# Bucket attention and two dense layers: the order of early loads and of two roundings

## What is computed

```python
q_bits = (einsum('bhsd,dk->bhsk', q, proj) > 0)      # the same for k
q_bucket = sum(q_bits * 2 ** arange(6))              # a bucket number for each row
mask = q_bucket[:, :, :, None] == k_bucket[:, :, None, :]
scores = where(mask, q @ k.T / 8, -1e9)
x = softmax(scores) @ v                              # then 1536 tokens x 512
h = x @ w_in;  g = P(h) / (Q(h) + 1e-6);  y = g @ w_out      # 512 -> 2048 -> 512
h = y @ w_in2; g = h * relu6(h + 3) / 6;  out = g @ w_out2   # 512 -> 2048 -> 512
```

## Time and profile before

| | |
|---|---|
| median of 3 runs | 822.86 us (822.78 to 823.11) |
| profiled execution | 823.14 us, its span 821.3 us |
| PE busy | 766.7 us (93% of the span) |
| DVE, ACT, POOL busy | 479.0, 439.6, 223.3 us |
| chain that ended last | PE 85%, DMA 4%, ACT 3%, SP's queue 3% |
| mean granted clock of PE | 0.981 |

### The profile page before, as it was taken

How to read it: one execution, slowest core, us unless ns; L and a number is a source line. 1 busy time by engine, 2 the same in 40 slices (tenths; PEclk the granted TensorE clock), 3 DMA queues, 4 the chain that set the end, 5 groups by cost and what they waited for, 6 DMA issues and landing times.

```text
span 821.3 us, 11268 instructions
## 1 busy us (share of the span) xinstructions
PE 766.7 (93%) x3712; PEld 592.8 (72%) x3712; DVE 479.0 (58%) x793; ACT 439.6 (54%) x783; POOL 223.3 (27%) x364
## 2 busy tenths in 40 slices
PE   2689996887979999999999999999999999999998
PEld 1466665554656668888888888888888888888886
DVE  3577764555756668888988899984221322232223
ACT  1567665465656668987766689884222122212221
POOL 1455664554746514430000024443000000000000
PEclk9999997989989999999999999999999999999999
DMA  5634334333322013330000013331000100000001
GB/s 121 150 91 122 93 88 99 94 88 87 82 70 67 1 27 91 90 103 0 0 0 0 0 39 97 97 103 52 1 0 1 51 0 0 0 37 15 1 1 51
DMA packets 35372, 43.31 MB, mean 53 GB/s; under 512 B 4480, under 2 KB 23680, under 8 KB 35328
## 3 DMA queue, kind: packets, MB, share of 16 engines
q1 hardware_dynamic: 34752, 42.32, 19.4%
q10 hardware_dynamic: 576, 0.43, 0.2%
HBM read 26.61 MB, written 3.15 MB: 36 GB/s over the span
## 4 chain that ended last, share of the span: by engine, by line
PE 85%; DMA 4%; ACT 3%; SPq 3%; issue 2%; DVE 2%; ACTq 0%; POOL 0%; POOLq 0%; DVEq 0%
PE y_ps L912 32%; PE h_ps L858 11%; PE h_ps L859 11%; PE h_ps L860 11%; PE o_ps L838 6%; PE t_ps L821 6%; PE s_ps L811 4%; PE s_ps L812 3%; SPq L287 2%; DMA k_cross<-q_cross 2%; ACT probs L442 2%; DMA w_raw<-in_moe_w_in 2%; ACT q_main L436 1%; PE p_ps L795 1%; DMA bit_col<-bit_row 1%
## 5 line engine op out<-in xcount | busy, mean ns | idle before, releaser
L858 PE MATMUL h_ps<-x_hi,slot 128*128 (+1 forms) x384 | 149.7, 390 | 0.0
L859 PE MATMUL h_ps<-x_lo,slot 128*128 (+1 forms) x384 | 149.4, 389 | 0.0
L860 PE MATMUL h_ps<-x_hi,slot 128*128 (+1 forms) x384 | 149.4, 389 | 0.0
L704 DVE SCALAR_TENSOR_TENSOR t_abs<-t_abs,h_ps 128x512 f32<-128x512 f32 x48 | 33.0, 688 | 187.2 <-ACT t_abs L514 187.2
L401 POOL TENSOR_TENSOR slot<-w_raw,slot 128x512 fp32r<-128x512 f32 x64 | 81.8, 1295 | 206.9 <-ACT slot L469 206.7
L514 ACT ACTIVATE t_abs<-h_ps,three_col 128x512 f32<-128x512 f32 x48 | 33.1, 690 | 191.9 <-PE h_ps L860 191.9
L912 PE MATMUL y_ps<-g_hi,slot 128*128 128x512 f32 x384 | 126.1, 389 | 0.0
L442 ACT ACTIVATE probs<-s_ps,exp_bias,exp_scale 128x768 f32<-128x768 f32 x96 | 95.1, 991 | 52.0 <-POOL exp_bias L388 51.3
L612 DVE TENSOR_REDUCE neg_max<-s_ps 128x1 f32<-128x768 f32 x96 | 91.6, 954 | 52.6 <-PE s_ps L812 52.5
L912 PE MATMUL y_ps<-slot,g_hi 128*128 128x512 f32 x384 | 118.3, 389 | 0.0
L811 PE MATMUL s_ps<-k_cross,q_cross 128*128 128x512 f32 x192 | 79.6, 414 | 32.4 <-ACT probs L442 28.3
(11 more groups left out here) (71 smaller groups left out, 1173.0 us busy)
## 6 DMA issues: line engine op xcount, KB each, us to landing
w_raw<-in_moe_w_in SPq DMA_DIRECT2D x32, 256.0 KB, 2.7
w_raw<-in_moe_w_out SPq DMA_DIRECT2D x32, 256.0 KB, 2.7
raw<-in_q SPq DMA_DIRECT2D x17, 192.0 KB, 3.2
v_nat<-in_v SPq DMA_DIRECT2D x16, 192.0 KB, 2.5
raw<-in_k SPq DMA_DIRECT2D x15, 192.0 KB, 3.4
k_main<-q_main SPq DMA_DIRECT2D x15, 192.0 KB, 2.6
k_cross<-q_main SPq DMA_DIRECT2D x15, 192.0 KB, 3.1
k_cross<-q_cross SPq DMA_DIRECT2D x15, 192.0 KB, 2.6
```

The source lines that it names most:

```text
L858: mm(h_ps[b][:, :], w_hi, x_hi[:, kt, cols], start=(kt == 0), stop=False)
L859: mm(h_ps[b][:, :], w_hi, x_lo[:, kt, cols], start=False, stop=False)
L860: last = mm(h_ps[b][:, :], w_lo, x_hi[:, kt, cols], start=False, stop=(kt == KT - 1))
```

## The change

It does four things. The early weights of a pair are asked for right behind `load_v`, ahead of `place_head`. They are split in steps 7 and 10 instead of 4 and 8. The projection weights are the first DMA of both queues. The second copy of head 0 goes to `swapped`, which is `probs[3]`, so that `raw[1][0]` is free: `load_raw(1, 0)` stands right behind the loads of the first pair, `load_raw(1, 1)` behind the first bits, ahead of `place_head(1)`, and `load_v(0)` behind that.

```diff
-    EARLY_AT = (4, 8)
+    EARLY_AT = (7, 10)
...
+            swapped = probs[3]
...
+            sp.dma_start(proj_raw[0:D, :], proj).then_inc(proj_in, 16)
             sp.dma_start(raw[0][0][0:D, :], q_dram[dram_head(0, 0), :, :]).then_inc(raw_in[0][0], 16)
-            sp.dma_start(raw[1][0][D:P, :], q_dram[dram_head(0, 0), :, :]).then_inc(swapped_in, 16)
-            sp.dma_start(proj_raw[D:P, :], proj).then_inc(proj_in, 16)
+            sp.dma_start(swapped[D:P, :], q_dram[dram_head(0, 0), :, :]).then_inc(swapped_in, 16)
             load_raw(0, 1)
+            load_raw(1, 0)
             sp.wait_ge(bits_made, 1)
             sp.wait_ge(first_q, 2)
             place_bits(sp, 0, 0)
+            load_raw(1, 1)
+            place_head(1)
             load_v(0)
-            place_head(1)
-            sp.wait_ge(first_k, 2)
-            load_raw(1, 0)
-            load_raw(1, 1)
             load_raw(2, 0)
             load_raw(2, 1)
...
                 if u == 0 and i >= 1:
                     load_v(i)
+                if u == 0 and EARLY_PAIR <= i < EARLY_PAIR + EARLY_SLOTS:
+                    load_weights(0, i - EARLY_PAIR)
                 if h + 2 < NHEAD:
                     place_head(h + 2)
                 if h + 6 < NHEAD:
                     load_raw((h + 6) // 2, h % 2)
-                if u == 0 and EARLY_PAIR <= i < EARLY_PAIR + EARLY_SLOTS:
-                    load_weights(0, i - EARLY_PAIR)
...
+            act.dma_start(proj_raw[D:P, :], proj).then_inc(proj_in, 16)
             act.dma_start(raw[0][0][D:P, :], k_dram[dram_head(0, 0), :, :]).then_inc(raw_in[0][0], 16)
-            act.dma_start(proj_raw[0:D, :], proj).then_inc(proj_in, 16)
-            act.dma_start(raw[1][0][0:D, :], k_dram[dram_head(0, 0), :, :]).then_inc(swapped_in, 16)
+            act.dma_start(swapped[0:D, :], k_dram[dram_head(0, 0), :, :]).then_inc(swapped_in, 16)
```

More of the change, by code:

```diff
@@ L489, in _ @@
             for to in (k_main, k_cross):
-                nc.scalar.activation(to[0][0:D, :], raw[1][0][0:D, :], ACT.Copy).then_inc(first_k, 1)
+                nc.scalar.activation(to[0][0:D, :], swapped[0:D, :], ACT.Copy).then_inc(first_k, 1)
             act.wait_ge(bits_made, 1)
@@ L661, in _ @@
             dve.wait_ge(swapped_in, 32)
-            nc.vector.tensor_copy(q_cross[0][D:P, :], raw[1][0][D:P, :]).then_inc(first_q, 1)
+            nc.vector.tensor_copy(q_cross[0][D:P, :], swapped[D:P, :]).then_inc(first_q, 1)
             nc.vector.tensor_tensor(q_cross[0][0:D, :], raw[0][0][0:D, :], q_main[0][0:D, :].bitcast(F32),
```

## The result

The changed kernel takes 786.82 us (median of 4 runs, 786.21 to 787.28) against 822.99 us (822.78 to 823.25) for the kernel before, a ratio of 0.956 with a 95% interval of 0.9543 to 0.9577. Its span is 785.5 us, 35.8 less than before. The prediction was 787.5 us, a gain of 35.4; the medians differ by 36.2.

What follows compares the result with a forecast made beforehand. PE bounds pair 2; the early pairs lose time to a weight wait and lower clock, the beginning to late loads. 30.9 - 4.1 + 8.6 = 35.4 us gained, from 822.86 to 787.5 us, range 782.5 to 793.0.

Steps and rivals of the forecast that it cites:

- -30.9 us: Attention pairs 3 to 6: asking for early weights first removes the whole wait and the clock's fall, -30.9 us.
- +1.02 x 4 = +4.1 us: Early pairs: POOL's split in step 8 delays exponential 9, costing PE 1.02 us in each of four pairs.
- the 0.2 assumed: Early pairs: ACT's own split delays exponential 7 by some 0.2 us, for which PE does not wait.
- The price of the split in step 11: Early pairs: POOL's second split, moved from step 9 to 11, costs nothing, as POOL idles after odd steps.
- The term of 8.6 us: Beginning: pair 1's loads in front bring scores 2 8.8 us earlier, less 0.2 for company beside bit_col.
- Projection weights first ... worth nothing by itself: Start of both queues: two tiny DMAs moved ahead of raw[0][0] gain nothing, since first bits wait for bit_col.
- the rule cited from the Trainium skill: Beginning: transfers from different engines share 16 DMA engines and interleave; by it alone the gain is 6.5 instead of 8.6 us.
- Rivals 1 to 5: Split 8 hidden 783.4 (0.12); splits dearer 792.6 (0.13); late beginning 790.8 (0.10); weights late 814.3 (0.03); placing late 825.3 (0.01).
- rival 3: Beginning gives only its lower bound, 5.3 us, as bit_col or the second raw is late: 790.8 us, chance 0.10.

Runs made afterwards that it cites:

- the run with step 10: The changed kernel with splits in steps 7 and 9, so POOL's stand in steps 8 and 10: 787.52 us, ratio 0.9582.
- the run behind the bits: The changed kernel with load_raw(1, 0) behind the first bits, right ahead of load_raw(1, 1): 787.71 us, ratio 0.9585.
- the beginning alone: The changed kernel with the old order of the early weights and splits in steps 4 and 8: 816.06 us, ratio 0.9927.

## Why the prediction was right

**The wait.** -30.9 us was right: the order alone gave 30.85. It came from windows of equal work, with and without the wait, which also held what the fall of the clock cost. That both halves of the edit remove it independently was not in the prediction, though its numbers were: weights asked for 16.4 us behind the seam and at work 19.9 behind it, against step 7 at 19.0.

**The splits.** The place and the mechanism were right, shown by the run that moves POOL's split alone out of step 8 (the price goes) and the run that moves ACT's alone out of step 7 (it stays). The term "+1.02 x 4 = +4.1 us" measured 27.92 against 30.85, so 2.93 us, or 0.73 a pair. The delay itself measured 0.89; I took an exponential's start to the scores as 1.21 us, but that was a row behind the stall, at the low clock, and here it is 127.30 - 126.16 = 1.14. And I left out the 0.14 that PE gets back at the next tile. That ACT's own split does not delay PE was right; exponential 7 starts 19.56 us behind the seam against 19.54 in pair 2 before, even less than the 0.2 assumed. The price of the split in step 11, nothing, was right. Its reason, "an odd step, where POOL afterwards idles", was too narrow, as the run with step 10 shows.

**The beginning.** The term of 8.6 us measured 7.87, of which 7.16 stand at scores 2. The difference, by its own steps: `bit_col` came 1.02 us later, not 0.2, and the first key bits let scores 0 begin 5.97 us behind the first bits instead of 5.25, which I did not have at all. Scores 0 so began 1.74 us later. 13.59 us lay between scores 0 and scores 2 before and 4.69 now, so the middle part gave 8.90, and 8.90 - 1.02 - 0.72 = 7.16. The step that failed is "Projection weights first ... worth nothing by itself". With them back in their old places, and the extra `raw` still beside `bit_col`, the first bits are at 8.69 us again; this is one profiled execution, but it lies outside the 9.12 to 9.83 us of the seven profiled kernels that have them first and `bit_col` in its old place. I had looked for the cause in the extra `raw`, of which the run behind the bits (9.12, against 9.25 to 9.83) shows at most a part. Why two transfers of 1.5 KB ahead of two tiles cost `bit_col` a microsecond stays open.

The 0.72 us lie in the landing of the key bits. The second half of them is issued by ACT 2.3 us behind the start of the first bits both before (at 11.0 us) and after (at 12.0), and scores 0 follow 2.9 us behind that issue before and 3.7 after. From first bits to scores 0 it took 5.79 to 6.02 us in the nine other profiled kernels with a `raw` load of pair 1 issued right behind the first bits, and 5.25 to 5.48 in the three that load v there. That fits other company in the DMA engines. It is also the one place where the rule cited from the Trainium skill, "DMA: Bandwidth & Descriptors", section "Issuing engines are not separate DMA queues", would bear on the trace: these bits are issued by ACT and the tiles by SP. The trace is in line with it but does not show it, as the load at that point was not tried alone.

**The clock in pair 0.** The remaining 0.71 us are in no term. The prediction put a change of clock only at scores 2. The fall near 47 us, which the kernel before has and the changed one has not, was missed; the earlier trace rows do not show it either, as they dip only from 123 us on. The runs speak for chance: the two kernels that keep the old beginning (steps alone, order alone) have no such fall and take 51.22 us from scores 2 to the seam of pair 2, just as the changed kernel does. Over all profiled kernels this stretch took from 50.0 to 52.9 us with the same work. So a gain of a microsecond at the beginning can't be read from the total. And it was luck that the total came as close as it did: the beginning gave 7.16 us where 8.6 were forecast, and the cheaper splits (1.2 us) and this fall (0.7) made up for it.

Rivals 1 to 5 did not come: the split in step 8 was not hidden, the second one was free, no early weight was late, and no placed head was waited for. Of rival 3 a part came: `bit_col` was late, and the beginning gave 7.16 us at scores 2 and 7.87 at the seam of pair 2, between its 5.3 and the forecast 8.6.

## What to carry to other kernels

A wait in the middle of a queue is a distance between asking and using, and here moving either end removed all of it or all but 0.8 us: before doing both, look at which end is free, as the second may only bring its own price. A moved instruction should be placed by what stands right behind it in its queue and whether that is awaited; here one step of POOL's queue, 8 or 9, decided 3 us, and a wait of ACT for something else (`upper_x`) covered another. Windows between equal marks of the program gave each term to some hundredths, where totals scatter by more than a microsecond.

## What was not expected of the hardware

With two transfers of 1.5 KB at the head of the queues instead of in third and second place, `bit_col` (0.5 KB a column) landed between 9.2 and 9.8 us in six profiled kernels, at 9.1 in a seventh without the extra `raw` beside it, and at 8.7 with them in their old places. Why is open.

PE's clock in pair 0 rose to its full 2.4 GHz at very different times in the ten kernels with a changed beginning, by the lengths of its matmuls: at 19 to 20 us in two, at 22 to 25 in five and at 28 to 29 in three. In two of the five (the beginning alone, and POOL in step 9) it fell to 1.2 GHz again for 6.8 us, and for 3.4 us in the kernel before; in none of the others did it fall between scores 2 and the seam of pair 2. In that stretch the two have the same instructions as the changed kernel. From scores 2 to the seam of pair 2 the two early ones took 50.0 and 50.4 us, the three without a fall in the middle group 51.2 to 51.7, the late ones 52.1 to 52.4 and the two with the fall 52.9. So the time goes with the clock, by up to 2.9 us; what sets the moment of the rise is not shown.
